# Loading the second product's weights and operands during the first product's last units, with lo parts in place and tile stores in two pieces

## The reference, cut to what matters

```python
x = moe(attention(q, k, v))                 # (8, 576, 512), stage a of the kernel
h = relu(x^T @ w_tok1) @ w_tok2             # stage b
u = x + h^T                                 # 4608 tokens x 512
out = u + relu(u @ w_ch1) @ w_ch2           # w_ch1 512 x 1536, w_ch2 1536 x 512
```

## Time and profile before

| | |
|---|---|
| time, three runs | 1324.32 us median (1323.87 to 1326.78) |
| the profiled execution's own time | 1324.95 us |
| its span | 1323.1 us |
| PE busy | 1226.0 us, 93% |
| DVE, ACT, POOL busy | 788.0, 502.0, 369.2 us |
| stage c (first product), from its first matmul to the second product's first | 708.1 to 1013.9 us |
| stage d (second product), to its last matmul | 1013.9 to 1317.9 us |

### The profile page before, as it was taken

How to read it: one execution, slowest core, us unless ns; L and a number is a source line. 1 busy time by engine, 2 the same in 40 slices (tenths; PEclk the granted TensorE clock), 3 DMA queues, 4 the chain that set the end, 5 groups by cost and what they waited for, 6 DMA issues and landing times.

```text
span 1323.1 us, 20482 instructions
## 1 busy us (share of the span) xinstructions
PE 1226.0 (93%) x7750; PEld 1185.1 (90%) x7750; DVE 788.0 (60%) x1204; ACT 502.0 (38%) x819; POOL 369.2 (28%) x223
## 2 busy tenths in 40 slices
PE   5899999999999999899999988889899399999998
PEld 5799999999999999798999988889898399999998
DVE  3866666676766675645554855547464175556554
ACT  3534333333324242424334644445453133233321
POOL 4443534352525343405520532324200000000000
PEclk9999999999999999999999989889999699999999
DMA  9921414242424200244456566655677988979884
GB/s 258 168 43 54 79 47 76 66 71 71 71 71 71 71 0 36 79 160 163 151 200 209 215 263 261 221 201 234 241 284 313 359 257 251 275 183 284 250 254 97
DMA packets 263551, 220.29 MB, mean 166 GB/s; under 512 B 196545, under 2 KB 235585, under 8 KB 256961
## 3 DMA queue, kind: packets, MB, share of 16 engines
q1 hardware_dynamic: 263488, 219.45, 54.4%
HBM read 130.55 MB, written 88.87 MB: 166 GB/s over the span
## 4 chain that ended last, share of the span: by engine, by line
PE 49%; DMA 13%; issue 13%; DVE 8%; POOL 6%; ACT 5%; SPq 5%; DVEq 0%; POOLq 0%; ACTq 0%
DMA g_scratch<-attention_staged 10%; PE bank L42 9%; PE bank L44 9%; PE bank L43 9%; PE bank L1158 6%; PE bank L1160 6%; PE bank L1159 6%; SPq L1593 3%; DMA qkv_u_left<-u_scratch 3%; PE bank L236 2%; POOL qkv_down_lo L1288 1%; DVE weights_fraction L605 1%; POOL z_z L770 1%; PE bank L918 1%; DVE tokens_cos L602 1%
## 5 line engine op out<-in xcount | busy, mean ns | idle before, releaser
L42 PE MATMUL bank<-weights_tok,z_z 128*128 128x288 f32 x576 | 175.1, 304 | 14.6 <-ACT z_z L455 9.2
L44 PE MATMUL bank<-weights_tok,z_z 128*128 128x288 f32 x576 | 171.1, 297 | 0.0
L43 PE MATMUL bank<-weights_tok,z_z 128*128 128x288 f32 x576 | 171.0, 297 | 0.0
L42 PEld LDWEIGHTS bank<-weights_tok,z_z 128*128 128x128 f32 x576 | 109.5, 190 | 18.1 <-ACT z_z L455 10.6
L43 PEld LDWEIGHTS bank<-weights_tok,z_z 128*128 128x128 f32 x576 | 109.5, 190 | 0.0
L44 PEld LDWEIGHTS bank<-weights_tok,z_z 128*128 128x128 f32 x576 | 109.3, 190 | 0.0
L1158 PE MATMUL bank<-z_g_hi,weights_down 128*128 128x384 f32 x240 | 82.5, 344 | 25.4 <-DVE bank L1682 25.4
L755 POOL TENSOR_TENSOR weights_rms_inverse<-weights_mean_squares,weights_minus_half 128x8 f32<-128x8 f32 x40 | 65.5, 1638 | 137.7 <-DVE weights_mean_squares L572 137.5
L770 POOL TENSOR_TENSOR z_z<-tokens_cos,z_z 128x512 fp32r<-128x512 f32 x32 | 51.8, 1618 | 177.3 <-ACT z_z L455 176.5
L1444 DVE TENSOR_TENSOR attention_staged<-attention_staged 128x384 f32<-128x384 f32 x36 | 30.8, 855 | 94.1 <-ACT attention_staged L1390 94.0
L462 ACT ACTIVATE weights_x_channel_major<-attention_u 128x288 fp32r<-128x288 f32 x64 | 28.4, 444 | 150.4 <-DVE attention_u L633 150.4
(11 more groups left out here) (225 smaller groups left out, 3670.1 us busy)
## 6 DMA issues: line engine op xcount, KB each, us to landing
g_scratch<-attention_staged SPq DMA_DIRECT2D x36, 1344.0 KB, 6.7
attention_raw_g<-g_scratch SPq DMA_DIRECT2D x20, 1152.0 KB, 9.1
tokens_raw_g<-g_scratch SPq DMA_DIRECT2D x11, 1152.0 KB, 8.7
z_raw_g<-g_scratch SPq DMA_DIRECT2D x11, 1152.0 KB, 9.4
weights_down<-w_scratch SPq DMA_DIRECT2D x7, 1536.0 KB, 14.9
x_scratch<-attention_u SPq DMA_DIRECT2D x8, 1152.0 KB, 4.2
u_scratch<-attention_u SPq DMA_DIRECT2D x8, 1152.0 KB, 6.2
weights_raw_u<-u_scratch SPq DMA_DIRECT2D x6, 1536.0 KB, 8.8
```

The lines of the kernel that those rows point to most:

```text
L42: eng.matmul(out, w[0], x[0], start=first, stop=False)
L43: eng.matmul(out, w[0], x[1], start=False, stop=False)
L44: return eng.matmul(out, w[1], x[0], start=False, stop=last)
```

## The change

Four things are changed together.

1. The tile store is split: five of the seven tiles (`PLACE` puts FIRST, SHARED, MIDDLE, THIRD, LATE in front) go after t3 (`store_early`, 960 KB), SECOND and LAST after t4 (`store_late`, 384 KB), with semaphores of their own. `w2_store` moves one unit back, and the second-product weights get a second hi buffer. ACT's SECOND relu waits for the late piece, all others for the early one.
2. w_ch1's seven combinations are laid out by unit (`up` is one tensor of [128, 6 units, 7 products, 2 parts, 2, 128]), so a unit's weights of all products lie side by side. Weights and operands of stage d are placed over them, and `ahead` loads them one after the other, from unit 30 on.
3. In stage d every product k has a raw operand tile of its own (seven), the lo part is written into it, and three hi slots stay. The next group's operand k is loaded when product k of this group is done.
4. The residual is loaded in two halves; each half of the next group is loaded within this group. The second use of the half (`take22`) is moved behind the fifth lo part in DVE's queue. Output stores wait on five semaphores in place of ten.

The core of the diff:

```diff
@@ phase_b
-            act.activation(wu[k][0][:, :, :], up_source(k)[:, :, :], ACT.Copy).then_inc(a_w, 1)
+            act.activation(up_part(k, 0), up_raw(k), ACT.Copy).then_inc(a_w, 1)
+    def up_part(k, h):
+        return wu[:, :, k, h, :, :].rearrange("p i t f -> p t i f")
...
+            gp.tensor_tensor(up_part(k, 1), up_raw(k), up_part(k, 0).bitcast(F32), ALU.subtract).then_inc(g_w, 1)
@@ phase_c
+PLACE = {FIRST: 0, SHARED: 1, MIDDLE: 2, THIRD: 3, LATE: 4, SECOND: 5, LAST: 6}
+EARLY = 5
...
     def w2_hi_step(act, s):
-        for i in range(4):
-            act.wait_ge(s_raw[i], DMA * (j + 1))
+        act.wait_ge(s_raw, 4 * DMA * (j + 1))
         wait(act, g_w2sum, w2_sums(s))
-        wait(act, s_w2, 2 * DMA * s)
+        wait(act, s_w2[s % 2], 2 * DMA * (s // 2))
...
+        if s > 0:
+            gp.wait_ge(s_w2[(s - 1) % 2], 2 * DMA * ((s + 1) // 2))
...
-    def store(sp, n):
+    def store_early(sp, n):
+        g, i = divmod(n, NI)
+        sp.wait_ge(d_t3, n + 1)
+        sp.dma_start(g_dram[g, :, i, 0:EARLY, :], staged[n % 2][:, 0:EARLY, :]).then_inc(s_early[n % 2], DMA)
+
+    def store_late(sp, n):
         g, i = divmod(n, NI)
         sp.wait_ge(d_t4, n + 1)
-        sp.dma_start(g_dram[g, :, i, :, :], staged[n % 2][:, :, :]).then_inc(s_g[n % 2], DMA)
+        sp.dma_start(g_dram[g, :, i, EARLY:NP, :], staged[n % 2][:, EARLY:NP, :]).then_inc(s_late[n % 2], DMA)
...
             if n >= 2:
-                store(sp, n - 2)
-            if n in W2_UNIT:
-                w2_store(sp, W2_UNIT[n])
-            if n == UNITS - NI + 2:
-                sp.wait_ge(p[LAST], n - 2)
-                sp.wait_ge(s_w2, 4 * DMA * NP)
-                nxt["load_first"](sp)
-        nxt["load_weights"](sp, range(1, 5))
-        store(sp, UNITS - 2)
-        nxt["load_weights"](sp, range(5, NP))
-        sp.wait_ge(s_g[0], DMA * UNITS // 2)
-        nxt["load_third"](sp)
-        store(sp, UNITS - 1)
+                store_late(sp, n - 2)
+            if n >= 1:
+                store_early(sp, n - 1)
+            if n - 1 in W2_UNIT:
+                w2_store(sp, W2_UNIT[n - 1])
+            if n == UNITS - NI:
+                for s in s_w2:
+                    sp.wait_ge(s, 2 * DMA * NP)
+            if n >= UNITS - NI:
+                nxt["ahead"](sp, i)
+        store_late(sp, UNITS - 2)
+        nxt["ahead"](sp, NI)
+        store_early(sp, UNITS - 1)
+        nxt["ahead"](sp, NI + 1)
+        store_late(sp, UNITS - 1)
@@ phase_d
+    def load_operand(sp, g, k):
+        wait(sp, p[k], NJ * g)
+        sp.dma_start(raw[k][:, :, :].bitcast(F32), g_dram[g, :, :, PLACE[k], :]).then_inc(s_g[k], DMA)
...
+    def ahead(sp, step):
+        last = prev["p"][LAST]
+        if step == 0:
+            load_operand(sp, 0, FIRST)
+        elif step == 1:
+            sp.wait_ge(prev["d_lo"], NP * NG)
+            load_weight(sp, FIRST)
+        elif step == 2:
+            sp.wait_ge(last, UNITS - 5)
+            load_operand(sp, 0, SHARED)
+        elif step == 3:
+            load_weight(sp, SHARED)
+        elif step == 4:
+            load_weight(sp, MIDDLE)
+        elif step == 5:
+            sp.wait_ge(last, UNITS - 3)
+            load_operand(sp, 0, MIDDLE)
+            load_weight(sp, SECOND)
+        elif step == 6:
+            for stored in prev["stored"][0]:
+                sp.wait_ge(*stored)
+            load_operand(sp, 0, SECOND)
+        else:
+            sp.wait_ge(prev["p"][MIDDLE], UNITS)
+            sp.wait_ge(prev["d_c22"], UNITS)
+            load_u2(sp, 0, 0)
...
-        dve.tensor_tensor(slot(M)[1][:, :, :], raw[M % NR][:, :, :], slot(M)[0][:, :, :].bitcast(F32),
+        dve.tensor_tensor(raw[k][:, :, :], raw[k][:, :, :].bitcast(F32), his[M % NH][:, :, :].bitcast(F32),
                           ALU.subtract).then_inc(d_lo, 1)
...
+        sp.wait_ge(last, UNITS - 1)
+        load_weight(sp, THIRD)
+        load_operand(sp, 0, THIRD)
+        load_u2(sp, 0, 1)
+        sp.wait_ge(last, UNITS)
+        load_operand(sp, 0, LATE)
+        load_weight(sp, LATE)
+        load_operand(sp, 0, LAST)
+        load_weight(sp, LAST)
         for g in range(NG):
             for k in range(NP):
-                M = NP * g + k
                 if g > 0 and k == 0:
                     store(sp, g - 1, 7)
-                    load_u2(sp, g)
-                if M + NR < TOTAL:
-                    load_operand(sp, M + NR)
+                if g + 1 < NG:
+                    load_operand(sp, g + 1, k)
+                    if k == MIDDLE:
+                        load_u2(sp, g + 1, 0)
                 for o in STORES.get(k, []):
                     store(sp, g, o)
+                if g + 1 < NG and k == LAST:
+                    load_u2(sp, g + 1, 1)
```

More of the change, by code:

```diff
@@ L1195, in slot, with tile @@
         return ub[(NP * g + k) % NS]
+    def tile(n, k):
+        return staged[n % 2][:, PLACE[k], :]
     def bank(i):
@@ L1343, in open_bank @@
         def open_bank(out):
-            pe.matmul(out, wu[FIRST][0][:, 0, 0:P], slot(0, FIRST)[0][:, 0, :], start=True, stop=True)
+            pe.matmul(out, wu[:, 0, FIRST, 0, 0, :], slot(0, FIRST)[0][:, 0, :], start=True, stop=True)
         def third(n):
@@ L1389, in relu @@
             act.wait_ge(*ready)
-            act.activation(staged[n % 2][:, k, :], src, ACT.Relu).then_inc(done, 1)
+            act.activation(tile(n, k), src, ACT.Relu).then_inc(done, 1)
         def relu21(n):
+            wait(act, s_late[n % 2], DMA * (n // 2))
             relu(n, SECOND, bank_f, (p[LAST], n + 1), a_g21)
@@ L1418, in scalar @@
                 act.activation(bank_f, bank_a(n - 1), ACT.Copy).then_inc(a_f, 1)
-                relu(n - 1, THIRD, staged[(n - 1) % 2][:, THIRD, :], (d_c22, n), a_g22)
+                relu(n - 1, THIRD, tile(n - 1, THIRD), (d_c22, n), a_g22)
             if n < UNITS:
@@ L1434, in t4 @@
         def t4(n):
-            st = staged[n % 2]
             dve.wait_ge(a_g21, n + 1)
             dve.wait_ge(d_t2, n + 1)
-            dve.tensor_tensor(st[:, LAST, :], st[:, SECOND, :], st[:, MIDDLE, :], ALU.subtract).then_inc(d_t4, 1)
+            dve.tensor_tensor(tile(n, LAST), tile(n, SECOND), tile(n, MIDDLE), ALU.subtract).then_inc(d_t4, 1)
         def t1(n):
-            st = staged[n % 2]
             dve.wait_ge(a_g11, n + 1)
             dve.wait_ge(a_g12, n + 1)
-            dve.tensor_tensor(st[:, SHARED, :], st[:, LATE, :], st[:, FIRST, :], ALU.subtract).then_inc(d_t1, 1)
+            dve.tensor_tensor(tile(n, SHARED), tile(n, LATE), tile(n, FIRST), ALU.subtract).then_inc(d_t1, 1)
         def c22(n):
             dve.wait_ge(a_f, n + 1)
-            wait(dve, s_g[n % 2], DMA * (n // 2))
-            dve.tensor_tensor(staged[n % 2][:, THIRD, :], bank_a(n), t5[n % 2][:, :], ALU.add).then_inc(d_c22, 1)
+            wait(dve, s_early[n % 2], DMA * (n // 2))
+            dve.tensor_tensor(tile(n, THIRD), bank_a(n), t5[n % 2][:, :], ALU.add).then_inc(d_c22, 1)
         def u4(n):
@@ L1568, in hi @@
         M = NP * g + k
-        act.wait_ge(s_q[M % NR], DMA * (M // NR + 1))
+        act.wait_ge(s_g[k], DMA * (g + 1))
         if M == 1:
-            act.wait_ge(prev["p"][FIRST], UNITS)
-        if M >= NS:
-            act.wait_ge(p[(M - NS) % NP], NJ * ((M - NS) // NP + 1))
-        act.activation(slot(M)[0][:, :, :], raw[M % NR][:, :, :], ACT.Copy).then_inc(a_hi, 1)
+            act.wait_ge(prev["p"][SECOND], UNITS)
+        if M == 2:
+            act.wait_ge(prev["p"][LATE], UNITS)
+        if M >= NH:
+            before = M - NH
+            act.wait_ge(p[before % NP], NJ * (before // NP + 1))
+        act.activation(his[M % NH][:, :, :], raw[k][:, :, :].bitcast(F32), ACT.Copy).then_inc(a_hi, 1)
     def lo(dve, g, k):
@@ L1590, in store @@
         sp.wait_ge(d_x, index + 1)
+        wait(sp, s_x[index % AHEAD], PARTS * DMA * (index // AHEAD))
         for part in range(PARTS):
@@ L1623, in product @@
         for t in range(FT):
-            wt, x = [w[:, h, j, t, :] for h in range(2)], [x[:, t, :] for x in slot(NP * g + k)]
+            wt, x = [w[:, h, j, t, :] for h in range(2)], [x[:, t, :] for x in (his[(NP * g + k) % NH], raw[k])]
             if onto:
```

136 lines of the change are left out of this document (63 added, 73 removed).

## The result

The changed kernel takes 1262.36 us (median of four runs, 1260.45 to 1263.44) against 1325.55 us for the kernel before, run beside it: ratio 0.952, 95% interval 0.9498 to 0.9542. The forecast was 1259, with 1244 to 1281 as its range. Run again later, the same kernel had 1263.76 us and a ratio of 0.9511.

The account below looks back on a forecast made before the run. TensorE's pace was taken as the bound, with 85.7 us lost in the two products to late seeds and a lower clock. Savings of 42.3, 12.7 and 10.9, 65.9 from 1324.95, gave 1259 us, range 1244 to 1281.

Parts of the forecast that it names:

- Part 1: First product: tile store in two pieces and weight store one unit later save 42.3 us; bounds 20 and 44.
- The cost of the split: Tile stores: 36 more transfers taken at no cost; bounds 0 and 1.35 us of queue time per piece.
- Rival (d): DMA queue: each piece holds it for its fixed 1.35 us, 8 us on both stalls' dates: 1267; chance 0.08.
- The serial reading of the 2.0 us: Tile stores: about 2.0 us fixed per transfer, if serial 2 us a unit; would make it 12 us and 1271.
- Part 2: Second product's first group: loads moved into the last six units; loss 16.8 us in place of 29.5, saved 12.7.
- Rival (e): SP's wait for unit 34's store: THIRD, LATE and LAST each stall some 5 us: 1274; chance 0.05.
- The second wait: Second product's first group: seed for LAST stands behind the next FIRST's lo part in VectorE's queue; stall 4.9 us.
- Part 3: Second product's later groups: residual in halves, loaded a group ahead, saves 10.9 us; bounds 5 and 11.4.
- no more than now: Second product: without the cover of early operand loads, each group would cost 38.8 us plus gaps, no more than before.
- Part 4: Stage before the first product: first weights laid out by unit cost 0; bound 3 us.
- Rival (f): TensorE without gaps for 560 us is granted a lower clock; at 0.85 the time is 1351; chance 0.02.
- The sum: Whole kernel: 42.3 + 12.7 + 10.9 = 65.9 us off 1324.95 gives 1259 us.

Follow-up runs that it names:

- Experiment 9: Tile store in one piece and weight store in its own unit together, against the changed kernel: 1298.34 us, ratio 0.9773.
- experiment 4: Tile store as one DMA after t4 again, against the changed kernel: 1276.46 us, ratio 0.9608.
- experiment 5: Weight store asked for in the unit of its step again, against the changed kernel: 1277.70 us, ratio 0.9607.
- Experiment 1: Residual's first half and unit 35's stores issued before SP's wait for unit 34's store, against the changed kernel: 1258.96 us, ratio 0.9483.
- experiment 2: Seeds for LAST and C22 sums before the next group's FIRST lo part in VectorE's queue, against the changed kernel: 1257.08 us, ratio 0.9467.
- Experiment 6: From the second group on, residual loaded behind the previous group's last output store, against the changed kernel: 1306.33 us, ratio 0.9828.
- experiment 8: Residual's first half before weight SECOND, against the kernel with SP's residual order and VectorE's seed order both changed (1250.76 us): 1252.99 us, ratio 0.9436.

## Why the prediction was right, and where it was off

**Part 1, right in place and nearly in size.** The tile store's late issue behind SP's wait for POOL was the cause, and 42.3 us were forecast from it and 44.7 came (44.8 lost before, 0.1 now). Experiment 9 brings the waits back. The forecast priced the split and the later weight store only as a pair, and did not see that either one alone leaves 14 to 16 us in the first product: with one piece, the store still comes too late behind loads (experiment 4), and with the wait for POOL, the early piece does (experiment 5). They are worth 36 us together and 21 or 22 each with the other undone (36 less 15 or 14), so there is no sense in giving each a share.

**The cost of the split, right.** 36 more transfers cost nothing that can be seen in the first product, whose stage runs at TensorE's pace. Rival (d), each piece holding the queue, was not needed: from 938.1 to 979.1, with late and early pieces among the loads, the queue moved 372 GB/s, 363 KB/us of the forecast's 370 (a KB is 1024 bytes), and the stage with 72 pieces has a loss of 0.1 us. The serial reading of the 2.0 us of the Trainium skill ("DMA: Bandwidth & Descriptors", Anatomy of one DMA) was not needed either. That section gives the figure for transfers that GpSimd issues; here SP issues all of them.

**Part 2, the step that was mis-sized: what SP's wait for unit 34's store costs.** It was forecast that the late piece would land at 56.8 on the clock of unit 30, that is at X + 11.0, and that the residual would be there 9.2 us later. SP's issues around it, X = 968.1:

```profile
965.86 0.32 SPq L1316 DMA_DIRECT2D g_scratch<-attention_staged  x1
966.22 0.87 SPq L1552 DMA_DIRECT2D weights_g<-g_scratch  x1
967.13 1.34 SPq L1555 DMA_DIRECT2D weights_down<-w_scratch  x1
968.52 0.54 SPq L1321 DMA_DIRECT2D g_scratch<-attention_staged  x1
982.54 0.53 SPq L1552 DMA_DIRECT2D attention_g<-g_scratch  x1
```

The piece landed at 982.5, X + 14.4, 3.4 us late. The queue's rate in the same stretch, 966 to 994 in 40 slices of 0.7 us (busy share in tenths, and GB/s):

```profile
DMA  9899989999999998932211000469999899999999
GB/s 307 325 435 428 395 327 384 384 417 454 467 408 437 410 410 338 355 140 88 110 75 53 26 0 0 53 147 298 380 290 204 215 424 432 439 382 419 408 413 518
```

Read the slices: 355 GB/s at 977.9, then 140, 88, 110, 75, 53, 26 and 0, until 298 again at 985. The bytes were nearly gone at 979, which is X + 11, the very date of the forecast (about 0.25 MB were left); so the rate of 370 KB/us was right. What failed is the step from "its bytes are moved" to "it has landed", which I took as nothing beyond the queue, and the step back to full rate, which I took as 1.4 us. The landing came 3.4 us late. The residual's half then landed at 993.8, 11.4 us behind the piece, where the forecast had 9.2: full rate took about 2.5 us to come back, 1.1 more than I took, and what the other 1.1 us are (slices of 290, 204 and 215 GB/s at 986 to 988, other loads served beside it) no run separates. With 0.2 us by which TensorE came earlier, these make the 5.8 us between the forecast wait, 6.9, and the measured 12.7. Experiment 1 confirms that the stop of the queue costs time: with the wait behind the residual the queue does not run dry and 3 to 4 us come back.

The trace also shows what the tail is. The landing of a transfer is counted there in sixteen steps, which I read as one for each of the 16 DMA engines. For unit 34's late piece twelve of them come from 977.9 to 978.5 and the last four at 980.8, 981.2, 981.8 and 982.5. The queue's row says the same: with a busy share of 0.34 falling to 0.06 and the rate falling in proportion (140 GB/s at 0.34, 26 at 0.06), a few engines still work at their usual rate and the others have nothing to do; packets in flight are 16 at 976.2, 4 at 979.0 and 1 at 981.8. The trace does not name the engines, but the pattern of twelve and four is the same in one transfer after another, well before the queue ran out. The last step came 0.1 us after the twelfth in the transfer that landed at 920.2, 2.0 at 939.3, 3.4 at 963.7 and 4.1 at 971.6. After the stop it was 0.4. In experiment 1, where the queue never stops, the piece lands just as late (X + 14.0). So the 3.4 us are not made by the stop: they are a lag that some four engines gathered while the queue was full, and whoever waits for a whole transfer waits for them. Why they lag is open.

Rival (e) named this wait of SP and gave it 15 us and a chance of 0.05. The wait did cost more than forecast, but the stalls of THIRD, LATE and LAST for their weights, from which its price was made, did not come.

**The second wait, right for its reason.** Forecast 4.9 us, measured 4.9. VectorE's queue is the cause (experiment 2). The data came 5 us later than forecast, 1021.5 or X + 53.4 in place of X + 48.2, but so did TensorE, so that the difference held. The chain there:

```profile
1001.19 20.34 DMA qkv_g<-g_scratch
1021.55 2.13 ACT tokens_g_hi L1608
...
1026.19 0.57 DVE bank L1747
1026.80 0.69 PE bank L1165
```

From 994 to 1021.5 the queue carried the forecast's 10368 KB in 27.5 us, where 28.0 was said. In sum the group lost 21.8 us and not 16.8, of it 17.6 in the two waits; the other 4.2 go to the lower clock in the main, where 4.6 was forecast for it.

**Part 3, right in size here.** The five waits are gone, and nothing of the 11.4 us is left. The remark that a group without the early operand loads would cost "no more than now" was not tested as it stands, for no run takes that cover away. Experiment 6 shows that the cover of the residual is worth 43 us, since the new operand buffers put 16 output stores, and with them the old place of the residual's load, behind a wait for the end of the group. The forecast did not have that price.

**Part 4, right.** POOL's lo writes in runs of 128 take 3514 ns on the mean of the four in this row, against 3515 before, and the stages ahead of the first product end at 707.0 after 708.1, which is within their spread:

```profile
L1115 POOL TENSOR_TENSOR weights_up<-z_raw_up,weights_up 128x1536 fp32r<-128x1536 f32 x4 | 14.0, 3514 | 64.7 <-ACT weights_up L1011 64.7
```

The lo part in place takes 2.56 us, as in the earlier trace rows. **Rival (f)**, a lower clock for a TensorE without gaps, did not come: 261 us at a granted clock of 1.00. No experiment undid part 4, the operand buffers or the in-place lo part by itself; that they cost nothing rests on these rows.

**The sum.** 64.5 us came off the span where 65.9 were forecast. The second product gave 19.1 and not 23.6 (12.7 and 10.9), 4.5 less, and 0.4 was lost behind it; the first product gave 2.4 more and the stages ahead 1.1. That the total came out so near is in part luck: the 4.5 us missing in the second product are offset by gains elsewhere, one of them mere spread. The profiled execution is thus 1.4 us over the forecast; the median of the four runs is some 2 us above that.

## What to carry to other kernels

In an in-order issuing queue look at what stands between a transfer that frees a buffer and the moment it is ready: a wait for another engine's result, asked for one step too early, cost 36 us here, and both a later request and a smaller, earlier piece were needed to cure it. Put no wait for a store's landing ahead of loads that don't need it when the queue is the bound, since the queue runs dry meanwhile and has to start again: 3 to 4 us here, all in all. Date a landing by the last DMA engine and not by the bytes: 3.4 us lay between the two here. And give the seed that the next product waits for its place before work for the next group, even when that work is usually ready.

## What the runs showed that had not been expected

Of 16 DMA engines, some four fell up to 4.1 us behind the others while the queue was full from 938 to 978, and a transfer's landing waits for the last of them: it came 4.5 us after the rate had collapsed at 978, in slices of 140 down to 0 GB/s, and 3.4 us after the date worked out from the bytes. Once the queue had stood still the lag was 0.4 us. Full rate took about 2.5 us to come back after the next issue. The Trainium skill ("DMA: Bandwidth & Descriptors", Queues, rings and completion order) says that the increment lands only after every earlier write of that engine; the late steps of the four engines would fit that, and no run here shows the share of that rule in it.

A small store among large loads lands when the bytes ahead of it have been moved: 12.3 us after its issue with 1920 KB of loads just ahead, 13.9 with 2688 (experiment 8). What stands behind it made no difference that can be seen (experiment 1).
